# Two pairs of weight sums move from GpSimd to VectorE, the first weights load later, and step 0's last products are put in another order

## The chip, the cores and the metric

The kernel runs on one core of a Trainium2 chip. The metric is the device time of one execution in microseconds. Before the change three runs took 817.11, 817.55 and 817.96 us (median 817.55).

## The reference, cut to what matters

Linear attention with a normalised output feeds two feed-forward layers:

```
kv  = einsum('bhsd,bhse->bhde', k, v)            # b=4, h=8, s=576, d=e=64
o   = einsum('bhsd,bhde->bhse', q, kv)
x   = o / sqrt(mean(o*o, -1) + 1e-6) * g_norm    # as tokens (2304) x features (512)
h   = x @ w_in;  x2  = (h * sigmoid(1.702*h)) @ w_out       # 512 -> 2048 -> 512
h2  = x2 @ w_in2; out = softplus(h2) @ w_out2               # 512 -> 2048 -> 512
```

## The kernel before, in words

**Attention.** Sixteen units, each one batch and one pair of heads (576 tokens), go through a chain that crosses three engines. For unit u TensorE makes the 64x64 key-value products (`kv_product`, L583), ScalarE copies them out of PSUM (`copy_kv`), TensorE makes the raw output (`raw_output`, L600 and L605), ScalarE squares it (`square`, L775), VectorE sums the squares (`sum_squares`, L980), ScalarE takes the root (L789), VectorE inverts it (L988) and multiplies (`scale`, L992, semaphore `scaled`), TensorE transposes (`turn`, L619, two units behind), and ScalarE writes the transposed tile with its gain into `xy` (L797, L800, semaphore `x_made`). Each engine takes these in one written order. `raw_output(u)` waits until unit u-2 is scaled, because two units share a pair of PSUM banks.

**The loads.** One queue, SyncE's, issues every large transfer: `load_kv` (L400), `load_q` (L410) and, at the units named in `W_AT`, `load_raw` (L419) for the raw weights of the up projection, 512 KB for one block of 256 hidden features. `load_q(u)` for u >= 6 and `load_kv(u)` for u >= 6 wait until a buffer is free.

**The feed-forward layers.** Tokens go in 3 chunks of 768, hidden features in 8 steps of 256, and there are two layers: 48 steps m. A step's up product is a 2x2 block product made with seven products instead of eight (the Winograd form): `P1, P6, P2, P7, P4, P5, P3` in this order. For it the weights need four sums S1 to S4 of their quarters (`w_sums`, L493 to L498, each 128x256) and the tokens need four sums T1 to T4 (`raw_x` on VectorE, L1011, each 128x768). Every operand is split into a rounded high part and a low rest, and each product is three matmuls over two blocks, six in all (L659). Product P1 uses the slot B11 of the tokens, P6 T2, P2 B21, P7 T3, P4 T4, P5 T1 and P3 B22. The splits of the first three weight blocks and of the first token chunk are GpSimd's, in one written order (L539 to L556): `w_sums(0)`, `w_high(0)` (L509), `w_low(0)` (L504), `x_early` (L534 the rounding, L536 the rest) for B11 and B21, then `w_sums(1)`, `w_high(1)`, `w_low(1)`, then the other token slots in the order of `X_EARLY`, then the first block of the down weights (L516, L522) and `w_sums(2)`.

**Step 0 lies inside the attention.** P1 of step 0 follows unit 10 on TensorE, P2 unit 12, P6 unit 14. After the last unit come P7, `turn(14)`, P4, P5, `turn(15)`, P1 of step 1, P3 of step 0. The products share two PSUM banks; VectorE adds them up (`add`, L1040: U2, U3, C21_ADD, C22_ADD, C12_ADD) and so forms the four tiles C11, C21, C22, C12 of the hidden features. ScalarE takes the sigmoid of a tile (L833), VectorE multiplies (`gate_product`, L1079) and splits the product (`gate_split`, L1085 and L1087; semaphore `g_split`). From step 1 on the down product of the step before (`down`, L732 and L735) is laid between the seven up products, in portions set by `shares`; its first matmul waits until tile C21 is split.

Of the kernel before, what the change touches and what calls it, by code (L numbers as in the profile page):

```python
# [42 lines left out]
A21 = S1  # L43
# [12 lines left out]
def build(nc, q_t, k_v, w_in1, w_out1, w_in2, w_out2, consts, out):  # L56
# [29 lines left out]
    with ExitStack() as ctx:  # L86
# [162 lines left out]
        def step_done(m):  # L249

            return max(products_done(m, k) for k in range(PRODUCTS))

# [30 lines left out]

        X_EARLY = (B11, B21, B22, T1, T3, T2, T4)
        X_EARLY_SUMS = (T1, T3, T2, T4)
# [110 lines left out]
        def _(sp):  # L396
# [15 lines left out]
            def load_raw(d):  # L412
                b = split_buffer(d)
                if d >= W_BUFS:
                    last = d - W_BUFS if d < STEPS else STEPS - W_BUFS if d == STEPS else None
                    if last is not None:
                        sp.wait_ge(prod_done, step_done(last))
# [29 lines left out]

            W_AT = {0: 0, 6: 1, 11: 2}
            load_kv(0)
# [37 lines left out]
        def _(pool):  # L487
            def w_sums(d):

                b = split_buffer(d)  # L490
                w32 = w_in32[:, b, LO]
                pool.wait_ge(w_in_landed[b], 16 * raw_loads(d))
                nc.gpsimd.tensor_tensor(w32[:, S3], w32[:, A11], w32[:, A21], ALU.subtract).then_inc(w_summed, 1)  # L493
                pool.wait_ge(w_summed, 4 * d + 1)
                nc.gpsimd.tensor_tensor(w32[:, S2], w32[:, A22], w32[:, S3], ALU.subtract).then_inc(w_summed, 1)
                nc.gpsimd.tensor_tensor(w32[:, S1], w32[:, A21], w32[:, A22], ALU.add).then_inc(w_summed, 1)
                pool.wait_ge(w_summed, 4 * d + 2)
                nc.gpsimd.tensor_tensor(w32[:, S4], w32[:, A12], w32[:, S2], ALU.subtract).then_inc(w_summed, 1)  # L498
                pool.wait_ge(w_summed, 4 * d + 4)

# [72 lines left out]
        def _(pe):  # L573
# [48 lines left out]
            def product(m, k):  # L622

                bank = bank_b(m) if k in (P6, P7, P4) else bank_a(m)
                new = k in (P1, P6, P5)
                if m % STEPS == 0:
                    if m == 0:
                        pe.wait_ge(x_split_early, X_EARLY.index(k) + 1)
                    else:
                        pe.wait_ge(x_split, x_splits(m // STEPS, k))  # L630
                if k == P1:
                    if m < STEPS:
                        pe.wait_ge(w_split, 7 * (m + 1))
                    else:
                        pe.wait_ge(w_in_landed[w_buffer(m)], 16 * operand_loads(m))
                    if m > 0:
                        pe.wait_ge(added, ADDS * (m - 1) + C21_ADD + 1)
                if k == P6 and m > 0:
                    pe.wait_ge(added, ADDS * (m - 1) + C12_ADD + 1)
                if k == P6 and m == 0:  # L640

                    pe.wait_ge(kv_copied, 2 * UNITS)
                if k == P2:
                    pe.wait_ge(t1_made, m + 1)
                if k == P7:
                    pe.wait_ge(added, ADDS * m + U2 + 1)
                if k == P4:
                    pe.wait_ge(added, ADDS * m + U3 + 1)
                if k == P5 and m == 0:
                    pe.wait_ge(c11_kept, 1)  # L650
                elif k == P5:
                    pe.wait_ge(hid_read, TILES * m + C11 + 1)
                if k == P3:
                    pe.wait_ge(added, ADDS * m + C22_ADD + 1)
# [99 lines left out]
            product(0, P4)  # L754
            product(0, P5)
            turn(UNITS - 1)
            product(1, P1)
            product(0, P3)
            for m in range(1, ALL):
                came = 0  # L760
                for k in range(PRODUCTS):
                    if (m, k) != (1, P1):
                        product(m, k)
                    down(m - 1, came, shares(m)[k])
# [5 lines left out]
        def _(act):  # L770
# [48 lines left out]
            def hidden(m, tile):  # L819
# [7 lines left out]
                else:  # L827
                    act.wait_ge(added, ADDS * m + (C21_ADD, C22_ADD, C12_ADD)[tile - 1] + 1)
                    h = hid(m, tile)
# [73 lines left out]
            for m in range(ALL):  # L903
# [3 lines left out]
                ends, begins = ends and not ends_late, begins and not begins_late  # L907
                if m > 0:
                    first_product(m)
# [38 lines left out]
                if begins:  # L948
                    copy_sums(ci - 1, 0, KT // 2 if ci < CHUNKS else 1)
                hidden(m, C22)  # L950
                if m in LATE_ROUNDS:
                    round_w_in(split_at(m))
# [16 lines left out]
        def _(dve):  # L969
# [26 lines left out]
            def raw_x(ci, slot):  # L996
# [21 lines left out]
            def add(m, which):  # L1018
# [13 lines left out]
                elif which == C22_ADD:  # L1032
                    dve.wait_ge(prod_done, products_done(m, P5))
                    dve.wait_ge(added, ADDS * m + U3 + 1)
                    to, bank, other = c22, a, c22
                else:
                    dve.wait_ge(prod_done, products_done(m, P3))
                    dve.wait_ge(added, ADDS * m + U2 + 1)
# [42 lines left out]

            def gate_split(m, tile):
                i = TILES * m + tile
                dve.wait_ge(hid_read, i + 1)
                nc.vector.tensor_copy(g_high(m, tile), hid(m, tile)).then_inc(g_hi_made, 1)  # L1085
                dve.wait_ge(g_hi_made, i + 1)
                nc.vector.tensor_tensor(g_low(m, tile), hid(m, tile), g_high(m, tile).bitcast(F32),  # L1087
# [22 lines left out]
            for m in range(ALL):  # L1110
# [5 lines left out]
                ahead = X_LATE_FROM <= ci + 1 < 2 * CHUNKS and p in (STEPS - 3, STEPS - 2)  # L1116
                if m == 1:
                    add(m, U2)
                if m > PHASE1:
                    softplus(m - 1, C12)  # L1120
                elif m > 0:
                    gate(m - 1, C12)
# [12 lines left out]
                if phase:  # L1135
                    add(m, U3)
                    softplus(m, C11)
                elif m > 0:
                    gate_product(m, C11)
# [11 lines left out]
                add(m, C21_ADD)  # L1151
                if m == 0:
                    gate_product(m, C11)
                if ends:
# [7 lines left out]
                add(m, C22_ADD)  # L1162
                if m == 0:
                    gate_split(m, C11)
                if phase:
# [82 lines left out]
```

## Time and profile before

| what | value |
|---|---|
| median of three runs | 817.55 us |
| the profiled execution | 817.59 us, of which the span of its instructions is 815.8 us |
| TensorE busy with matmuls | 804.6 us (99%) |
| VectorE, ScalarE, GpSimd busy | 589.9, 424.6, 225.4 us |
| granted TensorE clock | 1.000 over the span |

The span runs from the first to the last instruction of the profiled execution; 1.8 us of its own time lie around it. An engine's busy time is the union of its instructions; a record of the timeline starts when the engine takes up an instruction, so a stall inside the instruction lengthens it. In a timeline row the bracket at the end gives how long the engine was idle before it and what released it.

### The profile page before, as it was taken

To read this page: it belongs to the slowest core of one execution; us is meant where nothing else is said; L and a number is where in the kernel's file an instruction comes from. 1 tells how busy PE (TensorE), PEld (TensorE's weight loads), DVE (VectorE), ACT (ScalarE), POOL (GpSimd) and SP (SyncE) were. 2 spreads that over 40 slices of the span, in tenths; PEclk is the share of its full clock that TensorE was granted. 3 is DMA by queue.
4 is the path that set the end of the run, shared out by engine and by line. 5 is a ranking of instruction groups with operands and counts; after the bars stand their busy time and mean duration, and the time that the engine had idled before them with its cause. 6 is when DMAs were issued, how large, how long until landed. Compare 5 with 4: busy or idle time off the path is not lost.

```text
span 815.8 us, 12401 instructions
## 1 busy us (share of the span) xinstructions
PE 804.6 (99%) x4614; PEld 734.1 (90%) x4614; DVE 589.9 (72%) x1029; ACT 424.6 (52%) x809; POOL 225.4 (28%) x263
## 2 busy tenths in 40 slices
PE   8989999999999999999999999999999999999998
PEld 7878999999999999999998888888888988989886
DVE  3779767597665686666678777888767889766774
ACT  4762432333221233223247776688667678766765
POOL 4899987304421404264401401200000000000000
PEclk9999999999999999999999999999999999999999
DMA  9946537335455462666652535224433323442402
GB/s 356 406 168 238 205 142 291 149 116 218 167 210 198 162 234 91 244 219 233 221 188 95 206 109 206 100 90 158 163 119 121 151 91 101 162 178 90 147 35 78
DMA packets 24427, 139.80 MB, mean 171 GB/s; under 512 B 2224, under 2 KB 6960, under 8 KB 17200
## 3 DMA queue, kind: packets, MB, share of 16 engines
q1 hardware_dynamic: 24224, 138.95, 46.5%
q8 instruction: 37, 0.61, 0.3%
q14 instruction: 22, 0.18, 0.1%
q10 hardware_dynamic: 144, 0.07, 0.0%
HBM read 104.92 MB, written 34.08 MB: 170 GB/s over the span
## 4 chain that ended last, share of the span: by engine, by line
PE 92%; POOL 3%; DMA 1%; DVE 1%; ACT 1%; issue 1%; SPq 1%; ACTq 0%
PE ps L659 43%; PE ps L727 24%; PE ps L735 16%; PE ps L732 8%; DMA q_sb<-q_t 1%; POOL xs L536 1%; POOL xs L534 1%; POOL w_in L504 1%; PE ps L600 1%; SPq L400 0%; DVE gs_f L1040 0%; PE ps L619 0%; DVE ex L1096 0%; POOL w_in L509 0%; PE ps L583 0%
## 5 line engine op out<-in xcount | busy, mean ns | idle before, releaser
L659 PE MATMUL ps<-xs,w_in 128*128 128x384 f32 x2016 | 409.5, 338 | 2.5 <-POOL xs L536 1.7
L659 PEld LDWEIGHTS ps<-xs,w_in 128*128 128x128 f32 x2016 | 356.5, 188 | 27.5 <-POOL xs L536 1.9
L727 PE MATMUL ps<-w_out,gs 128*128 128x512 f32 x864 | 226.1, 393 | 0.0
L1040 DVE TENSOR_TENSOR gs_f<-ps,gs_f 128x384 f32<-128x384 f32 x240 | 133.2, 555 | 111.3 <-PE ps L659 109.7
L727 PEld LDWEIGHTS ps<-w_out,gs 128*128 128x128 f32 x864 | 160.0, 188 | 24.1 <-issue 0.5
L735 PE MATMUL ps<-gs,w_out 128*128 128x512 f32 x576 | 148.2, 392 | 0.0
L735 PEld LDWEIGHTS ps<-gs,w_out 128*128 128x128 f32 x576 | 105.6, 188 | 16.4
L504 POOL TENSOR_TENSOR w_in<-w_in_f,w_in 128x256 fp32r<-128x256 f32 x112 | 95.2, 887 | 28.8 <-ACT w_in L875 28.5
L833 ACT ACTIVATE lg<-gs_f 128x384 f32<-128x384 f32 x73 | 38.3, 525 | 122.4 <-DVE gs_f L1040 122.3
L732 PE MATMUL ps<-gs,w_out 128*128 128x256 f32 x576 | 83.9, 281 | 1.6 <-issue 1.6
L1107 DVE TENSOR_TENSOR gs<-gs_f,gs 128x384 fp32r<-128x384 f32 x96 | 55.4, 577 | 40.1 <-ACT gs L870 37.4
L870 ACT CAST gs<-gs_f 128x384 fp32r<-128x384 f32 x96 | 48.9, 509 | 67.4 <-DVE gs_f L1103 66.2
L732 PEld LDWEIGHTS ps<-gs,w_out 128*128 128x128 f32 x576 | 80.2, 188 | 1.8 <-issue 1.8
L522 POOL TENSOR_TENSOR w_out<-w_out_f,w_out 128x256 fp32r<-128x256 f32 x64 | 51.3, 834 | 96.2 <-ACT w_out L880 95.9
L1087 DVE TENSOR_TENSOR gs<-gs_f,gs 128x384 fp32r<-128x384 f32 x96 | 69.6, 725 | 3.3
L1096 DVE SCALAR_TENSOR_TENSOR ex<-fix,ex 128x384 f32<-128x384 f32 x96 | 54.0, 562 | 8.0 <-ACT fix L843 8.0
L1103 DVE TENSOR_TENSOR gs_f<-gs_f,ex 128x384 f32<-128x384 f32 x96 | 54.5, 568 | 3.3
L493 POOL TENSOR_TENSOR w_in_f<-w_in_f 128x256 f32<-128x256 f32 x16 | 12.4, 777 | 159.1 <-PE ps L659 94.8
L845 ACT ACTIVATE lg<-fix 128x384 f32<-128x384 f32 x96 | 50.5, 526 | 3.0
L841 ACT ACTIVATE ex<-ex 128x384 f32<-128x384 f32 x96 | 50.4, 525 | 3.0
L843 ACT ACTIVATE fix<-ex 128x384 f32<-128x384 f32 x96 | 50.4, 525 | 3.0
L839 ACT ACTIVATE ex<-gs_f 128x384 f32<-128x384 f32 x72 | 37.3, 519 | 27.6 <-DVE gs_f L1040 27.6
(64 smaller groups left out, 591.1 us busy)
## 6 DMA issues: line engine op xcount, KB each, us to landing
w_in<-w_kept SPq DMA_DIRECT2D x40, 1792.0 KB, 7.5
w_kept<-w_in SPq DMA_DIRECT2D x16, 1792.0 KB, 10.7
w_in_f<-w_in SPq DMA_DIRECT2D x16, 512.0 KB, 4.1
w_out_f<-w_out SPq DMA_DIRECT2D x16, 512.0 KB, 8.8
kv_in_sb<-k_v SPq DMA_DIRECT2D x8, 640.0 KB, 11.1
kv_in_sb<-k_v SPq DMA_DIRECT2D x8, 576.0 KB, 12.6
q_sb<-q_t SPq DMA_DIRECT2D x16, 288.0 KB, 11.0
out<-xy SPq DMA_DIRECT2D x18, 256.0 KB, 7.7
```

The source lines that it names most:

```text
L504: nc.gpsimd.tensor_tensor(w[:, LO, slot], w32[:, LO, slot], w[:, HI, slot].bitcast(F32), ALU.subtract).then_inc(w_split, 1)
L522: nc.gpsimd.tensor_tensor(w_out[:, f, LO, cols], w_out32[:, f, LO, cols], w_out[:, f, HI, cols].bitcast(F32), ALU.subtract).then_inc(w_out ...
L659: mm = nc.tensor.matmul(ps[:, bank, 0:HALF], w[:, wp, W_OF[k], cols], xs[:, k, xp, t], start=(new and t == 0 and (wp, xp) == (HI, HI)), st ...
L727: mm = nc.tensor.matmul(ps[:, acc_bank(1, j), 0:DM], g[:, j * P:(j + 1) * P], w, start=new, stop=done)
L732: mm = nc.tensor.matmul(half, w[:, j * P:(j + 1) * P], g[:, 0:NARROW], start=new and j % 2 == 0, stop=done, skip_group_check=True)
L735: mm = nc.tensor.matmul(ps[:, ACC_BANK + j, 0:WIDE], w[:, j * P:(j + 1) * P], g[:, NARROW:CHUNK], start=new, stop=done)
L845: nc.scalar.activation(lg[:, i % 2], fix[:, i % 2], ACT.Ln).then_inc(log_made, 1)
L1040: nc.vector.tensor_tensor(to, bank, other, ALU.add).then_inc(added, 1)
L1087: nc.vector.tensor_tensor(g_low(m, tile), hid(m, tile), g_high(m, tile).bitcast(F32), ALU.subtract).then_inc(g_split, 1)
L1096: nc.vector.scalar_tensor_tensor(out=ex[:, i % 2], in0=fix[:, i % 2], scalar=-1.0, in1=ex[:, i % 2], op0=ALU.add, op1=ALU.subtract).then_i ...
L1103: nc.vector.tensor_tensor(low, low, ex[:, i % 2], ALU.subtract).then_inc(soft_made, 1)
L1107: nc.vector.tensor_tensor(g_low(m, tile), hid(m, tile), g_high(m, tile).bitcast(F32), ALU.subtract).then_inc(g_split, 1)
```

## The change

The load of the first raw weights moves from behind unit 0's queries to behind unit 4's. The weight sums of blocks 0 and 1 become VectorE's, behind `scale(2)` and `scale(5)`; GpSimd starts with `x_early(B11)` and waits for the sums ahead of `w_high`. GpSimd's token order puts T1 last in place of second among the sums. In step 0 P5 comes ahead of P4 on TensorE, and P1 of step 1 goes behind P3 of step 0, in its ordinary place. VectorE's order in step 0 is written anew, with U2 of step 1 ahead of the gate of C22, and no portion of step 0's down product stands behind P1 and P6 of step 1.

```diff
         def products_done(m, k):
-            place = {P2: P6, P6: P2, P3: PRODUCTS}.get(k, k) if m == 0 else -1 if (m, k) == (1, P1) else k
+            place = {P2: P6, P6: P2, P5: P4, P4: P5}.get(k, k) if m == 0 else k
             return PRODUCTS * m + place + 1
...
+        def adds_done(m, which):
+            place = {C21_ADD: C22_ADD, C22_ADD: C21_ADD}.get(which, which) if m == 0 else which
+            return ADDS * m + place + 1
...
-        X_EARLY = (B11, B21, B22, T1, T3, T2, T4)
+        X_EARLY = (B11, B21, B22, T3, T2, T4, T1)
...
-            W_AT = {0: 0, 6: 1, 11: 2}
+            W_AT = {4: 0, 6: 1, 11: 2}
...
             def w_high(d):
                 b = split_buffer(d)
+                pool.wait_ge(w_summed, 4 * d + 4)
...
-            w_sums(0)
+            x_early(B11)
             w_high(0)
             w_low(0)
-            x_early(B11)
             x_early(B21)
-            w_sums(1)
             w_high(1)
             w_low(1)
...
                 part = (3, 5, 7, 13, 14, 19, 24)
+                if m == 1:
+                    part = (0, 0, 7, 13, 14, 19, 24)
...
+            product(0, P5)
             product(0, P4)
-            product(0, P5)
             turn(UNITS - 1)
-            product(1, P1)
             product(0, P3)
...
+            def w_sums(d):                                   # VectorE
+                w32 = w_in32[:, split_buffer(d), LO]
+                dve.wait_ge(w_in_landed[split_buffer(d)], 16 * raw_loads(d))
+                nc.vector.tensor_tensor(w32[:, S3], w32[:, A11], w32[:, A21], ALU.subtract).then_inc(w_summed, 1)
+                dve.wait_ge(w_summed, 4 * d + 1)
+                nc.vector.tensor_tensor(w32[:, S2], w32[:, A22], w32[:, S3], ALU.subtract).then_inc(w_summed, 1)
+                nc.vector.tensor_tensor(w32[:, S1], w32[:, A21], w32[:, A22], ALU.add).then_inc(w_summed, 1)
+                dve.wait_ge(w_summed, 4 * d + 2)
+                nc.vector.tensor_tensor(w32[:, S4], w32[:, A12], w32[:, S2], ALU.subtract).then_inc(w_summed, 1)
...
                 scale(u)
+                if u in (2, 5):
+                    w_sums(0 if u == 2 else 1)
...
+                if m == 0:
+                    add(0, C22_ADD)
+                    gate_product(0, C11)
+                    add(0, C21_ADD)
+                    gate_high(0, C11)
+                    add(0, C12_ADD)
+                    gate_low(0, C11)
+                    gate(0, C21)
+                    add(1, U2)
+                    gate(0, C22)
+                    continue
```

## Rows read from the trace of the kernel before

**Rows 1.** Windows: stretch, length, busy us of each engine, clock, DMA share, GB/s.

```profile
20.00:40.00 20.00, 19.82 (x258) 18.01 (x257) 14.39 (x24) 14.64 (x42) 17.20 (x18) 1.00 1.03 406
60.00:70.00 10.00, 8.45 (x55) 7.86 (x53) 9.79 (x14) 2.60 (x5) 8.38 (x10) 1.00 0.92 327
500.00:700.00 200.00, 200.00 (x991) 179.38 (x990) 160.86 (x294) 149.35 (x294) 4.47 (x5) 1.00 0.37 131
```

**Rows 2.** TensorE's waits, whole run: line, releaser: us in total, times, longest.

```profile
PE ps L659 <- POOL xs L536: 1.7, 1, 1.7
PE ps L732 <- issue: 1.6, 1, 1.6
PE ps L600 <- DMA q_sb<-q_t: 1.1, 1, 1.1
PE ps L659 <- DVE gs_f L1040: 0.5, 2, 0.3
```

**Rows 3.** TensorE's timeline: start, length, line, instruction, [idle before, releaser].

```profile
16.75 1.16 PE L600 MATMUL ps<-kv_sb,q_sb 128*128 128x128 f32 x8 [1.13 <-DMA q_sb<-q_t]
...
21.83 1.15 PE L600 MATMUL ps<-kv_sb,q_sb 128*128 128x128 f32 x8
...
26.41 0.80 PE L583 MATMUL ps<-kv_in_sb 128*64 128x64 f32 x20 [0.18 <-DMA kv_in_sb<-k_v]
...
29.97 1.16 PE L600 MATMUL ps<-kv_sb,q_sb 128*128 128x128 f32 x8
...
48.70 0.60 PE L619 MATMUL ps<-consts_sb,x_tok 128*128 128x128 f32 x4
50.98 1.31 PE L659 MATMUL ps<-xs,w_in 128*128 128x384 f32 x6 [1.69 <-POOL xs L536]
...
70.31 1.31 PE L659 MATMUL ps<-xs,w_in 128*128 128x384 f32 x6
```

**Rows 4.** VectorE's timeline for units 3 (first two) and 6.

```profile
19.13 0.82 DVE L980 TENSOR_REDUCE rms<-sq_sb 128x10 f32<-128x640 f32 x1 [1.56 <-ACT sq_sb L775]
...
20.86 0.82 DVE L992 TENSOR_TENSOR x_tok<-ps,rms 128x640 f32<-128x640 f32 x1
...
26.66 0.68 DVE L980 TENSOR_REDUCE rms<-sq_sb 128x8 f32<-128x512 f32 x1
...
28.29 0.69 DVE L992 TENSOR_TENSOR x_tok<-ps,rms 128x512 f32<-128x512 f32 x1
```

**Rows 5.** Queries of unit 4: the issue in SyncE's timeline.

```profile
6.69 0.43 SPq L410 DMA_DIRECT2D q_sb<-q_t  x1
```

**Rows 6.** The same transfer in the DMA view: size, us from issue to landing.

```profile
q_sb<-q_t SPq DMA_DIRECT2D x1, 288.0 KB, 12.2
```

**Rows 7.** GpSimd's timeline: first weight sum of block 0, then slot B11.

```profile
8.72 0.73 POOL L493 TENSOR_TENSOR w_in_f<-w_in_f 128x256 f32<-128x256 f32 x1 [7.78 <-DMA w_in_f<-w_in]
...
20.00 0.82 POOL L534 CAST xs<-xy 128x768 fp32r<-128x768 f32 x1 [1.69 <-ACT xy L800]
20.90 1.83 POOL L536 TENSOR_TENSOR xs<-xy,xs 128x768 fp32r<-128x768 f32 x1
```

**Rows 8.** GpSimd and VectorE instructions that overlap, from both timelines.

```profile
43.05 1.83 POOL L536 TENSOR_TENSOR xs<-xs_f,xs 128x768 fp32r<-128x768 f32 x1
44.37 1.32 DVE L1011 TENSOR_TENSOR xs_f<-xy,xs_f 128x768 f32<-128x768 f32 x1
...
62.56 1.69 POOL L509 CAST w_in<-w_in_f 128x1792 fp32r<-128x1792 f32 x1 [1.54 <-DVE gs L1087]
62.80 1.85 DVE L1079 TENSOR_TENSOR gs_f<-gs_f,lg 128x384 f32<-128x384 f32 x1
```

**Rows 9.** Line 1087 over the run: duration in ns, min/median/max.

```profile
L1087 DVE TENSOR_TENSOR gs<-gs_f,gs x96: 557/559/1046, 59.4 to 428.1; 128x384 fp32r<-128x384 f32 x96
```

**Rows 10.** VectorE's timeline: C21_ADD of step 0 and U3 of step 1.

```profile
57.31 0.56 DVE L1040 TENSOR_TENSOR gs_f<-ps,gs_f 128x384 f32<-128x384 f32 x1 [0.50 <-PE ps L659]
...
69.72 0.54 DVE L1040 TENSOR_TENSOR gs_f<-ps,gs_f 128x384 f32<-128x384 f32 x1
```

More of the change, by code:

```diff
@@ L243, in products_done @@
         def products_done(m, k):
-            place = {P2: P6, P6: P2, P3: PRODUCTS}.get(k, k) if m == 0 else -1 if (m, k) == (1, P1) else k
+            place = {P2: P6, P6: P2, P5: P4, P4: P5}.get(k, k) if m == 0 else k
             return PRODUCTS * m + place + 1
-        def step_done(m):
-            return max(products_done(m, k) for k in range(PRODUCTS))
+        def adds_done(m, which):
+            place = {C21_ADD: C22_ADD, C22_ADD: C21_ADD}.get(which, which) if m == 0 else which
+            return ADDS * m + place + 1
         def split_buffer(d):
@@ L416, in load_raw @@
                     if last is not None:
-                        sp.wait_ge(prod_done, step_done(last))
+                        sp.wait_ge(prod_done, PRODUCTS * (last + 1))
                     sp.wait_ge(w_stored, 16 * ((last if last is not None else d - 1) + 1))
@@ L498, in w_sums @@
                 nc.gpsimd.tensor_tensor(w32[:, S4], w32[:, A12], w32[:, S2], ALU.subtract).then_inc(w_summed, 1)
-                pool.wait_ge(w_summed, 4 * d + 4)
             def w_low(d):
@@ L636, in product @@
                     if m > 0:
-                        pe.wait_ge(added, ADDS * (m - 1) + C21_ADD + 1)
+                        pe.wait_ge(added, adds_done(m - 1, C21_ADD))
                 if k == P6 and m > 0:
-                    pe.wait_ge(added, ADDS * (m - 1) + C12_ADD + 1)
+                    pe.wait_ge(added, adds_done(m - 1, C12_ADD))
                 if k == P6 and m == 0:
@@ L645, in product @@
                 if k == P7:
-                    pe.wait_ge(added, ADDS * m + U2 + 1)
+                    pe.wait_ge(added, adds_done(m, U2))
                 if k == P4:
-                    pe.wait_ge(added, ADDS * m + U3 + 1)
+                    pe.wait_ge(added, adds_done(m, U3))
                 if k == P5 and m == 0:
@@ L653, in product @@
                 if k == P3:
-                    pe.wait_ge(added, ADDS * m + C22_ADD + 1)
+                    pe.wait_ge(added, adds_done(m, C22_ADD))
                 w = w_in[:, w_buffer(m)]
@@ L761, in _ @@
                 for k in range(PRODUCTS):
-                    if (m, k) != (1, P1):
-                        product(m, k)
+                    product(m, k)
                     down(m - 1, came, shares(m)[k])
@@ L827, in hidden @@
                 else:
-                    act.wait_ge(added, ADDS * m + (C21_ADD, C22_ADD, C12_ADD)[tile - 1] + 1)
+                    act.wait_ge(added, adds_done(m, (C21_ADD, C22_ADD, C12_ADD)[tile - 1]))
                     h = hid(m, tile)
@@ L907, in _ @@
                 ends, begins = ends and not ends_late, begins and not begins_late
-                if m > 0:
+                if m > 1:
                     first_product(m)
@@ L950, in _ @@
                 hidden(m, C22)
+                if m == 0:
+                    first_product(1)
                 if m in LATE_ROUNDS:
@@ L1033, in add @@
                     dve.wait_ge(prod_done, products_done(m, P5))
-                    dve.wait_ge(added, ADDS * m + U3 + 1)
+                    dve.wait_ge(added, adds_done(m, U3))
                     to, bank, other = c22, a, c22
@@ L1037, in add @@
                     dve.wait_ge(prod_done, products_done(m, P3))
-                    dve.wait_ge(added, ADDS * m + U2 + 1)
+                    dve.wait_ge(added, adds_done(m, U2))
                     to, bank, other = c12, a, c12
@@ L1082, in gate_split, with gate_high @@
             def gate_split(m, tile):
+                gate_high(m, tile)
+                gate_low(m, tile)
+            def gate_high(m, tile):
                 i = TILES * m + tile
@@ L1085, in gate_split, with gate_low @@
                 nc.vector.tensor_copy(g_high(m, tile), hid(m, tile)).then_inc(g_hi_made, 1)
-                dve.wait_ge(g_hi_made, i + 1)
+            def gate_low(m, tile):
+                dve.wait_ge(g_hi_made, TILES * m + tile + 1)
                 nc.vector.tensor_tensor(g_low(m, tile), hid(m, tile), g_high(m, tile).bitcast(F32),
@@ L1116, in _ @@
                 ahead = X_LATE_FROM <= ci + 1 < 2 * CHUNKS and p in (STEPS - 3, STEPS - 2)
-                if m == 1:
-                    add(m, U2)
+                if m == 0:
+                    add(0, C22_ADD)
[8 more added lines that the diff above has]
+                    continue
                 if m > PHASE1:
                     softplus(m - 1, C12)
-                elif m > 0:
+                else:
                     gate(m - 1, C12)
@@ L1137, in _ @@
                     softplus(m, C11)
-                elif m > 0:
+                else:
                     gate_product(m, C11)
@@ L1151, in _ @@
                 add(m, C21_ADD)
-                if m == 0:
-                    gate_product(m, C11)
                 if ends:
@@ L1162, in _ @@
                 add(m, C22_ADD)
-                if m == 0:
-                    gate_split(m, C11)
                 if phase:
```

## The prediction

> **What bounds the kernel now.** I read the windows first: from 70 us to the end TensorE has hardly a gap (200.00 busy us in a window of 200), the granted clock is 1.00 (the 2.4 GHz level) throughout, and the stretch from 60 to 70 us is the last of the middle with an idle share, 1.55 us [rows 1]. So the matmuls behind 70 us are a fixed block that starts when step 1 is under way; what happens before that moves the end one for one. Next I read TensorE's waits. Ahead of that block stand 1.7 us for GpSimd's split of slot T2 (it holds product P6 of step 0), 1.6 us ahead of the first down product, 1.1 us for the queries of unit 3 and 0.5 us for two adds of VectorE [rows 2]. Then the timelines, to see what else is nearly late. The "issue" ahead of the first down product is in truth a wait for `g_split`: VectorE runs without a pause from the add C21_ADD at 57.31 to the add U3 of step 1, which ends at 70.26 [rows 10], and TensorE starts P4 of step 1 at 70.31 [rows 3]. This 12.95 us queue of VectorE is the real bound of the passage into the block.
>
> In the attention the loop is as tight: unit 3 is scaled at 20.86 + 0.82 = 21.68 and `raw_output(5)`, which waits for it, starts at 21.83; unit 6 is scaled at 28.98 and `raw_output(8)` starts at 29.97 [rows 3, 4]. So VectorE has 0.15 us to spare on unit 3 and 1.0 us on unit 6. That is the cover under which the change puts its eight weight sums.
>
> **The change part by part. The load.** 512 KB at 406 GB/s [rows 1] take 1.3 us. Moved behind unit 4's queries, they let the transfers of units 2 to 4 land 1.3 us sooner, and the 1.13 us ahead of unit 3 [rows 3] goes. But the bytes ahead of later transfers are the same: the keys of unit 8 still come at 26.3, for which TensorE waits 0.18 us at 26.41 [rows 3]. Alone this part is worth 0.1 to 0.2 us. It fixes when the first weights land: the old landing of unit 4's queries, 6.69 + 12.2 = 18.9 [rows 5, 6], as the weights are now the last of the same bytes.
>
> **The first sums.** No row shows a VectorE tensor_tensor of 128x256 with both inputs in SBUF. One of 128x384 takes 0.557 us at best [rows 9]. Two rows give its price when GpSimd is busy: the VectorE instruction at 44.37 runs to 45.69, which is 0.81 us behind the end of GpSimd's at 44.88; the one at 62.80 runs to 64.65, 0.40 us behind the end of GpSimd's at 64.25 [rows 8]. It stands still until GpSimd's instruction has ended and then runs at 1.05 ns an element. For 256 elements this makes 0.28 us behind a GpSimd instruction and 0.28 + 0.15 = 0.43 us alone. The Trainium skill says the same in "SBUF — State Buffer", section "Who interferes with whom": an instruction of VectorE with two SBUF inputs and one of GpSimd that reads SBUF take turns under an exclusive lock. By that rule, the trace agrees with its 0.40 and 0.81 us. If the port were shared at half rate instead, a sum would take 2 x 0.28 + 0.15 = 0.7 us beside GpSimd and a set 2.5 us, and the sum below would end 1.3 us lower, at 819.8; the record at 62.80, 1.85 us long where half rate gives 0.95, speaks against it.
>
> GpSimd now begins with B11, which waits for unit 1's tile; with unit 3's raw output (and the turn behind it) 1.3 us sooner that starts at 20.00 - 1.3 = 18.7, 0.82 us for the rounding and then 1.82 us for the rest [rows 7]. VectorE, standing in `w_sums(0)` since unit 2 was scaled, gets its weights at 19.0. S3 waits for the rounding, until 19.5, and ends at 19.8. S2 waits for S3, and by then GpSimd's 1.82 us instruction holds the port, until 21.6; S2 ends at 21.9, S1 and S4 follow at 0.35 us each, to 22.4. Only now comes `sum_squares(3)`, which before started at 19.13 [rows 4]: 3.2 us later. ScalarE's gain work is no longer ahead of the root, which gives 0.3 us back. Unit 3 is scaled at 24.5 in place of 21.68, `raw_output(5)` starts at 24.6 in place of 21.83: +2.7 us, after the 0.15 us to spare. The 0.18 us wait at 26.41 goes: +2.5.
>
> **The second sums** stand between `scale(5)` and `sum_squares(6)`, which followed at once (26.66, no wait) [rows 4]. With everything 2.5 to 2.7 us late they begin at 29.4. GpSimd, whose `w_high(0)` could start only at 22.4, then is through with `w_low(0)` and starts B21: again one short and one long instruction. That is 0.6 + 1.9 + 2 x 0.35 = 3.2 us (alone 1.5; about 4 x (0.28 + 0.7) less overlaps, some 3.5, if each sum waits for a GpSimd instruction of 0.73 [rows 7]). Unit 6 is scaled 5.6 us late, less 1.0 us to spare: `raw_output(8)` is 4.6 us late, and so is everything up to `turn(12)`, since this stretch of TensorE has no gap.
>
> **GpSimd's relief.** Eight instructions of 0.73 us [rows 7] leave it, and T2 is split third of the sums' slots in place of fourth, T1 last. The last token sum, made at 45.69 before [rows 8], comes at 50.1; T2, T4 and T1 at 2.65 us each [rows 7] are ready at 52.7, 55.4 and 58.0. `turn(12)` ends at 49.3 + 4.6 = 53.9 [rows 3], so P6 starts at 53.9 against 50.98: the 1.69 us wait is gone and +2.9 remain. P5 takes the place of P4, waits for no add (0.3 us less) and starts at 55.98 + 2.6 = 58.6, T1 being there since 58.0.
>
> **The tail.** VectorE's queue starts with C22_ADD when P5 is done, at 57.31 + 2.6 = 59.9. It holds the same instructions up to U3 of step 1, in another order, plus a wait of 0.5 us for P3: 59.9 + 12.95 + 0.5 = 73.35, against 70.26 [rows 10]. P1, P6 and P2 of step 1 in one go before the down product fill the 1.55 us gap [rows 2], but TensorE then waits up to 2 us for U3. P4 of step 1 comes 3.1 us late; as VectorE meets GpSimd's last splits and `w_sums(2)` in other places, up to 0.9 us more. I take +3.5. The loads for block 3 on SyncE's queue now wait for P3 of step 0 and go out some 2 us later; that costs nothing, as block 3 stands behind all of `w_low(2)` on GpSimd.
>
> Sum: +2.7 - 0.2 + 2.1 - 1.7 - 0.3 + 0.5, and 0.4 for the tail: +3.5 us. The profiled execution took 817.59 (span 815.8 and 1.8 around it), which is the median of the runs to 0.04. **Forecast 821.1 us**; this case alone spans 819.5 to 823.2.
>
> **The rivals.**
>
> *The sums are cheap.* GpSimd's instructions miss them, each set costs 1.5 us: unit 3 is scaled 1 us late and unit 6 1.3 us late beyond that, less 1.0. Then TensorE reaches `turn(12)` 1.3 us late, P6's wait takes it up, and the tail is left at 0 to +1.5 us: 817.6 to 819.2, about 818.3. For it: alone a sum is 0.43 us. Against: B11 becomes ready within 0.3 us of the weights.
>
> *Faster: the sums lie in VectorE's pauses.* It decides at `sum_squares(3)`, which must start by 19.3, and at `sum_squares(6)`, by 27.5. For it: VectorE sits idle 1.56 us ahead of the first [rows 4]. Then the attention keeps its pace, P6 loses 1.69 us and the add's 0.3, and of the 1.55 us gap as much as VectorE's queue allows: between 817.6 - 1.0 = 816.6 (the queue still binds in full) and 817.6 - 3.5 = 814.1, say 815.5. Against: the weights land at 18.9, so four sums can't be through at 19.3.
>
> *Slower still: T1 holds P5.* T1 has 0.6 us to spare in my sum. If the rounding of block 0 or 1 waits longer for its sums, T1 is ready after 58.6 and VectorE's queue, too, starts later: 823 to 824.5.
>
> *The load does nothing*: the 1.3 us head start is lost again by unit 8 in any case; it is in the sum.
>
> **How the numbers follow.** Forecast case 0.58, cheap sums 0.20, faster 0.13, slower still 0.09. No change and a change can be told apart at 0.2%, 1.6 us: 815.9 and 819.2. Faster: 0.09 of the third case. Same: its other 0.04 and 0.16 of the cheap sums. Slower: 0.58 + 0.04 + 0.09 = 0.71. The range is 816.6 to 823.2; it leaves out the faster case's lower part and most of the slowest case.
>
> **What would show it.** In the changed kernel: `sum_squares(3)` at 22 us or later with two weight sums of 0.6 and 1.9 us ahead of it; a wait of TensorE of some 3 us ahead of `raw_output(5)` and of 2 us ahead of `raw_output(8)`, both released by VectorE's scaling; no wait of P6 for GpSimd; a wait of P4 of step 1 for the add U3; TensorE full from 74 us on. Wrong it would be if the weight sums take 0.43 us each and `raw_output(8)` starts before 31.5 us.

## The result

The changed kernel takes **823.91 us** (median of 6 runs, 822.34 to 824.46) against 818.01 us (6 runs, 817.11 to 818.13): ratio 1.0075, 95% interval [1.0064, 1.0085]. It is slower by 0.75%. The forecast was 821.1 us with a range of 816.6 to 823.2: the sign was right, the time 2.8 us too low and just outside the range. The profiled execution took 823.97 us, its span 822.2 against 815.8. Five of the six executions had a mean granted clock of 0.995 or 0.996 (823.57 to 824.46 us), the sixth 0.998 (822.34 us).

The changed kernel's windows, with the columns of [rows 1]:

```profile
20.00:40.00 20.00, 14.77 (x180) 13.23 (x180) 15.15 (x26) 10.65 (x29) 17.42 (x19) 0.91 1.03 406
70.00:80.00 10.00, 8.13 (x36) 7.20 (x35) 7.51 (x11) 1.66 (x3) 9.92 (x13) 0.83 0.35 128
500.00:700.00 200.00, 200.00 (x990) 179.26 (x989) 159.97 (x290) 146.96 (x287) 7.58 (x8) 1.00 0.35 124
```

Of 20 us TensorE works 14.77, not 19.82, and the granted clock, 1.00 everywhere before, is 0.91 and 0.83 in the two stretches with pauses. Its waits over the run, as in [rows 2]:

```profile
PE ps L600 <- DVE x_tok L995: 5.3, 3, 3.7
PE ps L659 <- DVE gs_f L1054: 2.3, 3, 1.9
```

The waits for the queries and for GpSimd's split are gone; in their place stand 7.6 us for VectorE. TensorE's timeline, as in [rows 3]:

```profile
24.80 2.05 PE L600 MATMUL ps<-kv_sb,q_sb 128*128 128x128 f32 x8 [3.66 <-DVE x_tok L995]
...
35.51 1.13 PE L600 MATMUL ps<-kv_sb,q_sb 128*128 128x128 f32 x8 [1.43 <-DVE x_tok L995]
...
54.37 1.30 PE L659 MATMUL ps<-xs,w_in 128*128 128x384 f32 x6
...
58.13 1.31 PE L659 MATMUL ps<-xs,w_in 128*128 128x384 f32 x6 [0.23 <-DVE gs_f L1054]
...
59.63 2.34 PE L659 MATMUL ps<-xs,w_in 128*128 128x384 f32 x12
...
75.25 2.17 PE L659 MATMUL ps<-xs,w_in 128*128 128x384 f32 x6 [1.87 <-DVE gs_f L1054]
...
78.07 1.55 PE L659 MATMUL ps<-xs,w_in 128*128 128x384 f32 x6
...
83.97 1.23 PE L659 MATMUL ps<-xs,w_in 128*128 128x384 f32 x6
```

`raw_output(5)` is +2.97 us late (24.80 against 21.83), `raw_output(8)` +5.54, P6 +3.39 (its wait for GpSimd is gone), P4 of step 1 +4.94. Behind the pauses of 3.66 and 1.87 us the same matmuls are slow: eight of 128x128 take 2.05 us in place of 1.15, P4 2.17 in place of 1.31. Behind the pause of 1.43 us they are not. Two more rows of the trace of before are needed, the start of P4 and P5 of step 0 (in the changed kernel P5 and P4, at 59.63) and P1 of step 2:

```profile
55.98 2.35 PE L659 MATMUL ps<-xs,w_in 128*128 128x384 f32 x12 [0.31 <-DVE gs_f L1040]
...
77.49 1.23 PE L659 MATMUL ps<-xs,w_in 128*128 128x384 f32 x6
```

P1 of step 2 is at 83.97 in place of 77.49: from P4 of step 1 to it 8.72 us in place of 7.18. From there on TensorE is full, and the span ends 6.4 us later.

VectorE's two sets of sums, each with the reduction that follows (compare [rows 4]):

```profile
18.73 0.42 DVE L1020 TENSOR_TENSOR w_in_f<-w_in_f 128x256 f32<-128x256 f32 x1 [1.11 <-DMA w_in_f<-w_in]
19.19 1.01 DVE L1022 TENSOR_TENSOR w_in_f<-w_in_f 128x256 f32<-128x256 f32 x1
20.12 2.03 DVE L1023 TENSOR_TENSOR w_in_f<-w_in_f 128x256 f32<-128x256 f32 x1
22.07 0.41 DVE L1025 TENSOR_TENSOR w_in_f<-w_in_f 128x256 f32<-128x256 f32 x1
22.41 0.80 DVE L983 TENSOR_REDUCE rms<-sq_sb 128x10 f32<-128x640 f32 x1
...
30.94 1.40 DVE L1020 TENSOR_TENSOR w_in_f<-w_in_f 128x256 f32<-128x256 f32 x1
32.37 0.42 DVE L1022 TENSOR_TENSOR w_in_f<-w_in_f 128x256 f32<-128x256 f32 x1
...
33.39 0.68 DVE L983 TENSOR_REDUCE rms<-sq_sb 128x8 f32<-128x512 f32 x1
```

and GpSimd's split of B11 and B21 beside them (compare [rows 7]):

```profile
19.09 0.82 POOL L536 CAST xs<-xy 128x768 fp32r<-128x768 f32 x1 [18.15 <-ACT xy L801]
20.00 1.87 POOL L538 TENSOR_TENSOR xs<-xy,xs 128x768 fp32r<-128x768 f32 x1
...
30.25 1.81 POOL L538 TENSOR_TENSOR xs<-xy,xs 128x768 fp32r<-128x768 f32 x1
```

A sum takes 0.42 us by itself. The one at 19.19 ends at 20.20, 0.29 us behind the end of GpSimd's rounding; the one at 20.12 ends at 22.15, 0.28 us behind the end of the 1.87 us instruction; the one at 30.94 ends at 32.34, 0.28 us behind the end of GpSimd's at 32.06.

### The profile page after: what moved, and what is told of

It reads as the page before. It is cut to its first block, busy times and chain, and to the rows that moved or that the text cites. A ratio compares the mean times of both kernels' runs of the same rounds, so it can differ in the third digit from the quotient of the medians.

```text
span 822.2 us, 12388 instructions
## 1 busy us (share of the span) xinstructions
PE 808.2 (98%) x4614; PEld 737.5 (90%) x4614; DVE 598.7 (73%) x1037; ACT 424.5 (52%) x809; POOL 214.9 (26%) x255
## 4 chain that ended last, share of the span: by engine, by line
PE 90%; DVE 5%; ACT 2%; DMA 1%; issue 1%; SPq 1%; ACTq 0%; DVEq 0%
PE ps L659 42%; PE ps L727 24%; PE ps L735 15%; PE ps L732 8%; DMA w_in_f<-w_in 1%; DVE xs_f L1014 1%; DVE rms L983 1%; DVE gs_f L1095 1%; DVE gs_f L1054 0%; SPq L401 0%; ACT rms L790 0%; DVE gs L1109 0%; DVE gs L1105 0%; SPq L411 0%; PE ps L600 0%
## 5 line engine op out<-in xcount | busy, mean ns | idle before, releaser
L504 POOL TENSOR_TENSOR w_in<-w_in_f,w_in 128x256 fp32r<-128x256 f32 x112 | 92.5, 861 | 28.6 <-ACT w_in L876 28.3
L1105 DVE CAST gs<-gs_f 128x384 fp32r<-128x384 f32 x96 | 52.9, 551 | 2.5
L1095 DVE TENSOR_TENSOR gs_f<-gs_f,lg 128x384 f32<-128x384 f32 x73 | 52.0, 712 | 0.1
```

The source lines that it names most:

```text
L504: nc.gpsimd.tensor_tensor(w[:, LO, slot], w32[:, LO, slot], w[:, HI, slot].bitcast(F32), ALU.subtract).then_inc(w_split, 1)
L1095: nc.vector.tensor_tensor(hid(m, tile), hidden_of(m, tile), lg[:, i % 2], ALU.mult).then_inc(hid_read, 1)
```

## The experiments

Twelve kernels. The question was first which part costs, then why the parts add up to more than their own waits, then whether a part is worth keeping. Each ratio compares a kernel with executions of the kernel before that were timed beside it; their medians lay between 817.47 and 818.01 us. Edits are against the changed kernel unless a text says otherwise, and cut to what matters.

**The tail alone.** All of the third part, the load and the sums as before:

```diff
-            W_AT = {4: 0, 6: 1, 11: 2}
+            W_AT = {0: 0, 6: 1, 11: 2}
-            x_early(B11)
+            w_sums(0)                      # GpSimd's, as before
             w_high(0)
             w_low(0)
+            x_early(B11)
             x_early(B21)
+            w_sums(1)
...
-                if u in (2, 5):            # VectorE's sums go
-                    w_sums(0 if u == 2 else 1)
```

> Only the third part of the change: T1 split last, P5 ahead of P4, P1 of step 1 behind P3, VectorE's new order in step 0. The load and both pairs of weight sums are as before. My theory (the loss is the VectorE sums that stand still behind GpSimd, plus TensorE's lower clock behind the long pauses): the attention keeps its times, raw_output(5) at 21.8 and raw_output(8) at 30.0; P6 no longer waits; C22_ADD starts near 55.5, but VectorE's queue up to U3 of step 1 is 14.2 us long as in the changed kernel and not 12.95, so P4 of step 1 starts at 69.7 and the time is 817.4, within 1 us of before (818.0). Rival (the new order of the tail is itself what costs): 819.5 or more, with a pause over 1.8 us ahead of P4 of step 1 and a clock below 1.00 there.

817.82 us (10 runs, 817.13 to 819.42) against 817.74 (13 runs), ratio 1.0003 [0.9994, 1.0013]. Nothing is gained. Six executions took 817.1 to 817.9 us, the other four 818.8 to 819.4 at a mean granted clock of 0.997 to 0.998. The profiled one is of these four; its TensorE timeline:

```profile
70.20 1.58 PE L661 MATMUL ps<-xs,w_in 128*128 128x384 f32 x6 [1.87 <-DVE gs_f L1056]
...
72.43 2.12 PE L661 MATMUL ps<-xs,w_in 128*128 128x384 f32 x6
...
78.92 1.23 PE L661 MATMUL ps<-xs,w_in 128*128 128x384 f32 x6
```

The pause and the 8.72 us behind it (70.20 to 78.92) are those of the changed kernel, without any weight sum on VectorE. VectorE's queue from C22_ADD to U3 takes 14.23 us here (55.91 to 70.14), as in the changed kernel (60.96 to 75.19).

**The sums alone.** Against the kernel before: the load and the sums moved, GpSimd's B11 first, the tail as before:

```diff
+            W_AT = {4: 0, 6: 1, 11: 2}
+            x_early(B11)                   # GpSimd, ahead of w_high(0)
+                if u in (2, 5):            # VectorE, behind scale(u)
+                    w_sums(0 if u == 2 else 1)
```

> The first two parts alone: the later load and both sets of sums on VectorE, with GpSimd starting at B11; token order, products and VectorE's order in step 0 as before. My theory: raw_output(5) at 24.8 behind a pause of 3.7 us, matmuls of 0.51 us in place of 0.29 behind it, raw_output(8) at 35.5; then VectorE's queue of 12.95 us, no pause over 1.7 us ahead of P4 of step 1 and no drop of the clock there: P4 of step 1 at 73.9, time 821.6, that is 2.3 us faster than the whole change. Rival (the attention alone explains the loss and the tail is neutral): 823.9 as the whole change. Second rival (tail order is the loss): 818 to 819.

821.83 us (4 runs), ratio 1.0046 [1.0029, 1.0063]. TensorE's timeline:

```profile
74.67 1.31 PE L657 MATMUL ps<-xs,w_in 128*128 128x384 f32 x6
```

P4 of step 1 is +4.36 us late, without a pause and at full clock. By the ratios the two parts alone make +3.8 us (0.46%) and nothing; together they make +6.1 (0.75%). Of the 2.3 us between, the rows show 2.1: P4 of step 1 is at 75.25 in place of 74.67 (0.58), and there the clock falls (1.54). These are two single executions. The one of the sums alone is the slowest of its four, and in its attention the clock stayed low for longer (0.50 from 24 to 30 us; in the changed kernel it was up again at 28).

**The pause filled.** The tail alone, with multiplications by zero in TensorE's order (the trace has two records for each of them):

```diff
+                    if (m, k) == (1, P4):
+                        fill(7)            # 7 matmuls of 128 zero columns into a bank that is cleared later
                     product(m, k)
```

> tail_only with seven extra matmuls of zeros by zeros ahead of P4 of step 1, added into an accumulator bank (they change nothing) while TensorE waits for U3. They fill 1.75 of the 1.87 us pause. In tail_only the executions fell in two groups, about 817.3 (mean clock 1.000) and 819.1 (0.998). My theory (the second group is the granted clock falling behind this pause): with the pause filled only the first group is left, all runs near 817.4, clock 1.00 from 70 to 80 us, and from P4 to P1 of step 2 7.2 us in place of 8.7. Rival (the two groups have another cause): two groups 1.7 us apart as before.

817.15 us (10 runs, 816.76 to 818.30), 0.9999 [0.9989, 1.0009]; every execution has a clock of 0.999 or 1.000. The group at the lower clock is gone, which four of ten against none of ten might still be by chance; the trace:

```profile
67.47 1.72 PE L674 MATMUL ps<-ex 128*128 128x128 f32 x14
69.53 1.31 PE L661 MATMUL ps<-xs,w_in 128*128 128x384 f32 x6 [0.34 <-DVE gs_f L1065]
...
76.71 1.23 PE L661 MATMUL ps<-xs,w_in 128*128 128x384 f32 x6
```

7.18 us from P4 to P1 of step 2. The same edit in the changed kernel, nothing else:

> The changed kernel with seven multiplications by zero of 128 columns ahead of P4 of step 1 and nothing else. The clock theory: TensorE no longer stands for 1.87 us there, P4(1) keeps its start at 75.2 and runs at full clock, so that P1(2) starts at 82.4 instead of 83.97 and the total is 822.1 to 822.6 (823.91 less the 1.54 us between 8.72 and 7.18). The rival, that the 8.72 us behind P4(1) have another cause, such as waits for splits or for PSUM that the records place on TensorE: 823.6 to 824.2.

```profile
73.32 1.73 PE L672 MATMUL ps<-ex 128*128 128x128 f32 x14
75.36 1.31 PE L659 MATMUL ps<-xs,w_in 128*128 128x384 f32 x6 [0.30 <-DVE gs_f L1063]
...
82.53 1.23 PE L659 MATMUL ps<-xs,w_in 128*128 128x384 f32 x6
```

P4 starts no earlier (75.36), yet P1 of step 2 is 1.44 us earlier. That is the clock, shown by one edit that takes no work away. The total is 822.97 us (5 runs, 822.53 to 823.48), 0.94 below 823.91 where 1.3 to 1.8 were expected; the two ratios, 1.0071 [1.0057, 1.0084] and 1.0075 [1.0064, 1.0085], cannot be told apart. The mechanism is settled by the trace; its size on the median is not.

**The first pause filled.** The changed kernel with 13 multiplications of zeros, into a bank that is free there, ahead of `raw_output(5)`:

```diff
+                if u == 5:
+                    zeros(13)
                 raw_output(u)
```

> The changed kernel with 13 extra matmuls on TensorE between the key-value product of unit 6 and raw_output(5), on a bank that is free; their results are thrown away. They fill 3.2 of the 3.7 us pause and wait for nothing. My theory (the pause is paid a second time through the granted clock): raw_output(5) starts at 24.8 as in the changed kernel, but the clock stays 1.00 from 20 to 40 us, its matmuls take 0.29 us, the key-value product of unit 7 starts at 26.9 in place of 28.2, and the time is 1.3 us lower, 822.6. Rival (a pause costs its own length only): the same 823.9, or more by whatever the extra matmuls delay.

A miss: 823.85 us (4 runs), 1.0077 [1.0062, 1.0092].

```profile
25.44 1.13 PE L600 MATMUL ps<-kv_sb,q_sb 128*128 128x128 f32 x8 [0.33 <-DVE x_tok L997]
...
35.50 1.13 PE L600 MATMUL ps<-kv_sb,q_sb 128*128 128x128 f32 x8 [2.14 <-DVE x_tok L997]
```

VectorE's timeline, the first sum of the first set and two of the second set:

```profile
19.58 0.91 DVE L1022 TENSOR_TENSOR w_in_f<-w_in_f 128x256 f32<-128x256 f32 x1 [2.35 <-DMA w_in_f<-w_in]
...
30.25 0.59 DVE L1022 TENSOR_TENSOR w_in_f<-w_in_f 128x256 f32<-128x256 f32 x1
30.87 1.92 DVE L1024 TENSOR_TENSOR w_in_f<-w_in_f 128x256 f32<-128x256 f32 x1
```

The clock is full now behind the first pause, but `raw_output(8)` starts where it did, at 35.50. Two things add up to this. In this execution the first weights landed 0.85 us later (19.58 against 18.73), and `raw_output(5)` came 0.64 us later (25.44). And the second set met GpSimd's split of B21 with a sum of 1.92 us, so that it took 3.1 us in place of 2.45. From `raw_output(5)` to `raw_output(8)` it is 10.06 us in place of 10.71: of the 1.33 us that the low clock had cost here, 0.65 came back and the rest went into the longer second set. The median shows nothing of either.

**GpSimd's weights first.** To keep the 1.87 us instruction away from the first set:

```diff
-            x_early(B11)
             w_high(0)
             w_low(0)
+            x_early(B11)
```

> The changed kernel with one difference: GpSimd splits block 0's weights ahead of slot B11, so that it is idle while VectorE makes the first four sums. My theory (a VectorE instruction with two SBUF inputs stands still until GpSimd's is over): the four sums take 0.43 us each, 18.7 to 20.2; sum_squares(3) starts at 20.2 in place of 22.4, raw_output(5) at 22.6 in place of 24.8 behind a pause of some 1.5 us, no drop of the clock behind it. The second set still meets GpSimd. Time 3.5 us below the changed kernel, 820.4. Rival (VectorE's sums are slow by themselves, or wait for the landing of the weights): first set as before, 22.4, and 823.9.

A miss, and slower: 825.79 us (4 runs), 1.0093 [1.0078, 1.0108]. The first set is cured, `raw_output(5)` is at 22.90. But B11, moved back, now meets the second set; VectorE's timeline:

```profile
19.02 0.42 DVE L1020 TENSOR_TENSOR w_in_f<-w_in_f 128x256 f32<-128x256 f32 x1 [1.41 <-DMA w_in_f<-w_in]
...
27.71 0.59 DVE L1020 TENSOR_TENSOR w_in_f<-w_in_f 128x256 f32<-128x256 f32 x1
28.34 1.92 DVE L1022 TENSOR_TENSOR w_in_f<-w_in_f 128x256 f32<-128x256 f32 x1
30.18 1.04 DVE L1023 TENSOR_TENSOR w_in_f<-w_in_f 128x256 f32<-128x256 f32 x1
31.14 2.02 DVE L1025 TENSOR_TENSOR w_in_f<-w_in_f 128x256 f32<-128x256 f32 x1
```

and TensorE's:

```profile
35.19 2.04 PE L600 MATMUL ps<-kv_sb,q_sb 128*128 128x128 f32 x8 [4.37 <-DVE x_tok L995]
```

One pause of 4.37 us in place of 3.66 and 1.43, with the clock low behind it and no second set left to absorb that. The clock falls once more ahead of P4 of step 1, behind a pause of 1.88 us: from P4 (77.68) to P1 of step 2 (86.42) it is 8.74 us. I had followed the moved instruction to the place it left and not to the place it came to.

**Both sets clear of it.** The same, with the second set behind unit 7:

```diff
-                if u in (2, 5):
+                if u in (2, 7):
```

> The changed kernel with both sets of VectorE's weight sums out of GpSimd's way: GpSimd splits block 0's weights ahead of B11, and the second set stands behind scale(7) in place of scale(5), when GpSimd has done B21. My theory (the sums cost what they stand still behind GpSimd): each set takes 1.5 us, all eight sums 0.42 us; raw_output(5) at 22.9, raw_output(8) near 31.2, turn(12) ends near 50.8, no clock drop in the attention; C22_ADD near 58.5, P4 of step 1 near 72.8 and, with the lower clock behind it in some executions, 820.3 to 821.8, that is 2 to 3.5 us below the changed kernel. Rival (any work put into VectorE's chain costs its length several times over, wherever GpSimd is): 823.5 or more.

820.64 us (5 runs), 1.0041 [1.0028, 1.0054]: 3.3 us better than the changed kernel, with the same eight sums on the same engine. All eight take 0.41 to 0.43 us; here is the sixth in VectorE's timeline, and then TensorE's rows for units 5 and 8, for P6, and for P4 of step 1 and P1 of step 2:

```profile
33.09 0.42 DVE L1022 TENSOR_TENSOR w_in_f<-w_in_f 128x256 f32<-128x256 f32 x1
```

```profile
22.75 1.13 PE L600 MATMUL ps<-kv_sb,q_sb 128*128 128x128 f32 x8 [1.47 <-DVE x_tok L995]
...
30.60 1.16 PE L600 MATMUL ps<-kv_sb,q_sb 128*128 128x128 f32 x8
...
51.90 1.31 PE L659 MATMUL ps<-xs,w_in 128*128 128x384 f32 x6 [1.68 <-POOL xs L538]
...
73.24 1.34 PE L659 MATMUL ps<-xs,w_in 128*128 128x384 f32 x6 [1.90 <-DVE gs_f L1054]
...
80.45 1.23 PE L659 MATMUL ps<-xs,w_in 128*128 128x384 f32 x6
```

`raw_output(8)` is +0.63 us late in place of +5.54. But P4 of step 1 is still +2.93 late, only 2.0 us better than in the changed kernel: the later second set holds GpSimd's `w_high(1)` until 34.24 (30.73 before), and P6 waits 1.68 us for the split of T2 again. The other 1.5 us of the gain are the clock, which in this execution did not fall behind the 1.90 us ahead of P4 (7.21 us to P1 of step 2). Four of the five executions took 820.22 to 820.98 us at 0.999 or 1.000, the fifth 822.65 at 0.998.

**VectorE's queue.** The tail alone, with one instruction put into a wait: `gate_low(0, C11)` ahead of the add that waits 0.69 us for P3.

```diff
                     gate_high(0, C11)
-                    add(0, C12_ADD)
                     gate_low(0, C11)
+                    add(0, C12_ADD)
```

> tail_only with one exchange in VectorE's order of step 0: the low split of C11 ahead of the add C12_ADD, which waited 0.69 us for product P3 with the split behind it. My theory (VectorE's queue up to U3 sets P4 of step 1): the wait is filled, the queue 0.5 us shorter, P4 of step 1 at 69.7, the pause ahead of it 1.4 us and so no drop of the clock: 816.9 in all executions, 0.9 below before. Rival (the queue's length is set by GpSimd's instructions, with which each gate takes turns, so that a filled wait comes back as a longer collision): 817.4 with two groups.

816.66 us (10 runs, 816.00 to 818.03), 0.9993 [0.9984, 1.0003]; the queue takes 13.35 us (14.23 without the edit). With six zero products ahead of P4 as well:

> tail_gl with six multiplications by zero of 128 columns in TensorE's order ahead of P4 of step 1, into a bank that the next first product clears. The clock theory: the pause of 1.76 us ahead of P4(1) shrinks to some 1 us and no execution shows a clock below 0.999, so that all lie within 815.9 to 816.9 and the median is 816.5 (tail_gl 816.66, tail_fill 817.15 against 817.74 without its filler). The rival, that tail_gl's scatter has another cause: executions at 817.9 and above come as often as before, median 816.7 to 817.2, and the products of zeros only make P4(1) later by up to 0.2 us.

816.75 us (11 runs, 815.88 to 817.42), 0.9993 [0.9984, 1.0002]; all clocks 0.999 or 1.000, and none of the 11 above 817.5. The one execution of ten at 818.03 us and a clock of 0.998 has no counterpart, but the median stays, inside the rival's 816.7 to 817.2, and five executions lie above the 816.9 that the theory allowed. These two are the best versions found, 0.7 to 0.8 us under the kernel before, which these runs cannot tell from no change.

**GpSimd's copy held back.** In the queue VectorE stands behind GpSimd's 1.7 us copy of block 2's weights [rows 8]. The tail alone, with this copy waiting until step 0's gates are split:

```diff
-            pool.wait_ge(g_split, C21 + 1)
+            pool.wait_ge(g_split, C12 + 1)
             w_high(2)
```

> tail_only with GpSimd held back: it starts the split of block 2's weights when tile C12 of step 0 is split, in place of tile C21. My theory (the 14.2 us queue of VectorE in step 0 holds some 3 us of standing still behind GpSimd): the product of C22 takes 0.55 us in place of 1.76, the splits 0.36 and 0.56 in place of 0.78 and 0.98; U3 of step 1 ends near 67, P4 of step 1 starts at 68.4 without a pause, no drop of the clock, and the time is 815.8, 1.9 us below before. Block 2 is then split by 74 to 75 us, ahead of P1 of step 2 at 75.6. Rival (GpSimd's split becomes the last thing P1 of step 2 waits for): a wait of P1 of step 2 for GpSimd of 1 to 3 us, 817 to 819.

A miss: 821.03 us (4 runs), 1.0044 [1.0029, 1.0059]. U3 ended 2.9 us sooner than in the tail alone and P4 started at 68.42 with no pause; then TensorE waited 3.51 us for GpSimd's split of the down weights, and the clock fell behind that: from the down product at 80.26 to P4 of step 2 at 90.72 it took 10.46 us, where the trace of before has 7.57 (78.56 to 86.13), 2.9 us more. Repaired twice, both on top of `gate_low` moved: release one gate earlier and the down weights ahead of block 3's sums,

```diff
-            pool.wait_ge(g_split, C21 + 1)
+            pool.wait_ge(g_split, C22 + 1)
-                if d:
+                if d and m > 1:
                     w_sums(d)
                 for pair, layer in w_out_of(m):
                     w_out_low(pair, layer)
+                if d and m == 1:
+                    w_sums(d)
```

> tail_gl with GpSimd's copy of block 2's weights held back until the third gate of step 0 is split (g_split 3), and with the down weights of pair 1 split ahead of block 3's sums, so that the first down product of step 1 does not wait as it did in tail_hold. Theory: U3(1) ends at about 68.9 (its steps no longer beside the 1.8 us copy), P4(1) starts by 69.1 against 69.74 in tail_gl, the first down product of step 1 at about 77.4 without a wait, total 815.9 to 816.2. Rival: block 3's sums, now 3 us later, hold ScalarE's copy of its weights and the logarithm behind it; the gate of C22 in step 1 then comes at 81 instead of 78.4 us and TensorE waits at a down product near 82 by 1 to 2 us: 817.5 or more.

819.18 us (7 runs), 1.0023 [1.0012, 1.0035]: the rival held, TensorE waited 1.91 us for ScalarE. Then ScalarE's copy of block 3 was moved behind the work that it held up:

```diff
-            LATE_ROUNDS = (1, STEPS)
+            LATE_ROUNDS = (STEPS,)
...
+                if m == 2:
+                    round_w_in(split_at(1))
...
-                if split_at(m) and m not in LATE_ROUNDS:
+                if split_at(m) and m != 1 and m not in LATE_ROUNDS:
```

> tail_hold_out with ScalarE's copy of block 3's weights moved behind the logarithm of C12 in step 1 and the copy of C11 of step 2, so that neither waits for block 3's sums. Theory (TensorE's 1.91 us at the third first product of step 2 came from that copy alone): P4(1) at 68.0, no wait above 0.7 us up to 90 us, every later product 1.5 to 1.8 us ahead of tail_gl; total 814.9 to 815.6, faster than before by 0.2 to 0.3%. Rival: block 3's splits on GpSimd still start at 80.4, and the first product of step 3, 1.7 us earlier now at 84.1, waits for them: 816 to 817.

819.19 us (11 runs), 1.0018 [1.0010, 1.0027], a miss again. P4 started at 67.83 and the first product of step 3 at 83.65, 2.1 us ahead of the best version; then

```profile
94.06 1.30 PE L736 MATMUL ps<-gs,w_out 128*128 128x256 f32 x9 [2.09 <-DVE gs L1113]
...
100.10 1.31 PE L663 MATMUL ps<-xs,w_in 128*128 128x384 f32 x6 [1.23 <-DVE gs_f L1060]
```

VectorE had stood for ScalarE, and ScalarE, one step back in its timeline, for GpSimd's sums of block 4:

```profile
88.94 1.70 ACT L880 CAST w_in<-w_in_f 128x1792 fp32r<-128x1792 f32 x1 [7.04 <-POOL w_in_f L499]
```

Three times the wait came back one place further on. The windows show what is full there. This kernel, from 62 to 82 us:

```profile
62.00:82.00 20.00, 19.63 (x120) 18.27 (x119) 17.13 (x26) 6.50 (x9) 16.57 (x19) 1.00 0.71 270
```

The best version (`gate_low` ahead of the add), the same stretch and the next:

```profile
62.00:82.00 20.00, 18.20 (x107) 16.43 (x106) 18.47 (x25) 5.18 (x7) 19.70 (x22) 1.00 0.61 234
82.00:102.00 20.00, 20.00 (x117) 18.70 (x116) 14.93 (x21) 8.10 (x10) 19.84 (x25) 1.00 0.50 187
```

GpSimd is busy 19.70 and 19.84 of 20 us there (19.21 and 19.69 in the kernel before). In the last kernel it is 3.1 us less busy from 62 to 82 us: it stands 1.47 us for the hold, at 62.2 to 63.7, and 1.81 us, at 78.9 to 80.7, for ScalarE's copy of block 3, which comes later since the down weights stand ahead of block 3's sums. Block 4's sums then end 1.7 us later than in the best version (88.91 against 87.21), and the total is 2.5 us above it. TensorE's lead at P4 is worth only what GpSimd can follow.

## Why the prediction was right in sign and short in size

**Right: the mechanism.** VectorE was the tight engine at both places, its sums stood behind GpSimd's long instructions (which of the four stood was off: I had the first behind the rounding and the second behind the long instruction, and it was the second and the third), `sum_squares(3)` started at 22.41 (22.4 forecast), `raw_output(5)` at 24.80 (24.6), P6's wait for GpSimd went, P4 of step 1 waited for U3. That 22.4 was hit so closely is in part luck: other sums stood than I had it, and my own terms, 21.9 and twice 0.35, add up to 22.6. The exclusive turn, with 0.28 us left of a 256-element sum behind the end of GpSimd's instruction, held to 0.01 us three times; half-rate sharing is out, as the sum at 20.12 took 2.03 us where that would give 0.7. The Trainium skill's rule in "SBUF — State Buffer", section "Who interferes with whom", that the two take turns under an exclusive lock, agrees with these rows. The run with both sets clear of it shows what this turn costs: nearly all of the delay at `raw_output(8)` (+0.63 in place of +5.54), and 2.0 of the 4.9 us at P4 of step 1. Of its 3.3 us in the total, 1.5 are the clock and not the turn. The cheap sums (818.3) and the sums in VectorE's pauses (815.5) are refuted. T1 never held P5: its split ended at 59.17, P5 started at 59.63. The rival built on it gave 823 to 824.5, the measured time, by a cause that did not occur.

**Wrong: the sum, by three terms.**

*The clock, priced at nothing; this is the step that failed.* The sum "+2.7 − 0.2 + 2.1 − 1.7 − 0.3 + 0.5, and 0.4 for the tail" counts a pause of TensorE at its own length. My text read the granted clock as 1.00 throughout before, and never asked what it would be behind a pause of 2 or 3 us, though it forecast both pauses. At P4 of step 1, with nothing behind it that waits, this costs 1.54 us of span in the profiled execution (8.72 against 7.18); the fillers, in two kernels, bring back 7.18 and 7.17. The stretch took 8.72 to 8.76 us in the four profiles in which the clock fell there, and 7.10 to 7.21 in the other ten. In the attention the pause of 3.66 us costs 1.33 us up to the next `kv_product` (24.80 to 28.20, against 21.83 to 23.90), and the second set starts as much later; half of that, 0.65 us, came back with the filler ahead of `raw_output(5)`, the other half is hidden by the second set.

*VectorE's queue in its new order.* Forecast 12.95 + 0.5, and 0.4 for the meetings with GpSimd; measured 14.23, from C22_ADD at 60.96 to the end of U3 at 75.19, +1.28. The tail alone has 14.23 too, and with both sets of sums clear of GpSimd it is 14.59. 0.69 of it is the wait for P3, and the `gate_low` edit takes 0.88 back.

*The start of the queue.* Forecast +2.6 for P5, measured +3.65 (59.63 against 55.98). `raw_output(8)` is late by 5.54 in place of 4.6: unit 5's scaling ended at 31.02, so that the second set, itself only 2.45 us long in place of 3.2, began at 30.94 in place of 29.4. That scaling ended 6.22 us behind the start of `raw_output(5)` where it was 4.92 before and 4.89 with the pause filled, so the late start is mostly the clock again. At P6 0.5 us of it is left (+3.39 in place of +2.9). Further, P6's result was added only behind unit 14's scaling, and P7 waited for that add (0.23 at 58.13): P7 is +4.19 late where P6 is +3.39. I had followed TensorE and GpSimd through this stretch, and not VectorE.

From 3.5 this makes 3.5 + 1.05 + 0.4 + 1.54 = 6.5 us for P1 of step 2, measured 6.48. Without the last term it would have been 822.5, inside my range. These terms are read from one profiled execution; on the medians the clock's part is open, as the run with the pause filled shows.

**What stays open.** Why the clock fell in four of ten executions of the tail alone and in the others did not is not explained by anything in the records. How much the load alone gives was not measured by itself. Nor was the changed kernel run with all of its pauses filled, which would give the clock's whole part.

## What to carry to other kernels

When a forecast holds a new pause of TensorE of about 2 us or more with full work behind it, price the pause and then, as something that may happen, the slow matmuls after it: here 1.3 and 1.5 us more in the changed kernel and 2.9 in the run with GpSimd held back. A few multiplications by zero in the pause kept the clock up. Before small instructions of VectorE are laid beside GpSimd, list GpSimd's long instructions at both places, the one that the change leaves and the one it comes to. And see which engine is at 98% over the stretch behind the wait that you remove: that is where the gain goes.

## What the hardware showed that I had not expected

- The granted clock fell to its lower level (1.2 GHz) behind pauses of TensorE of 1.87 (two profiles), 1.88 (two), 3.51, 3.57, 3.66, 3.70 and 4.37 us, and stayed at 2.4 GHz behind 1.43, 1.46, 1.47, 1.68, 1.76, 1.90, 1.91, 2.09 and 2.14 us. The length of the pause alone does not decide it: 1.87 us was enough in one profile, 2.14 us was not in another. In the tail alone the executions of one kernel fall into two groups some 1.6 us apart, with mean clocks of 0.997 to 0.998 and of 0.999 to 1.000; that the pause of 1.87 us is what parts them is seen in one profile and inferred for the rest.
- Multiplications by zero in the pause kept the clock up: it stayed at 0.999 or above in 21 executions of two kernels, and at 1.00 behind the filled pause in the profiles of two more.
- A VectorE instruction that needs 0.42 us was recorded at up to 2.03 us beside a GpSimd instruction of 1.87 us.
